# First head: one ScalarE table for squares and roots, centroids on ScalarE's queue, two wide copies of them, products of ones on TensorE meanwhile

## What is computed

```python
q_n = q / (norm(q) + 1e-6);  k_n = k / (norm(k) + 1e-6);  c_n = centroids / (norm(centroids) + 1e-6)
q_assign = argmax(einsum('bhsd,hcd->bhsc', q_n, c_n));  k_assign = argmax(einsum('bhsd,hcd->bhsc', k_n, c_n))
mask = q_assign[..., None] == k_assign[..., None, :]
scores = where(mask, q @ k.T / sqrt(64), -1e9)
attn = exp(scores - max) / (sum + 1e-9);  x = attn @ v
```

## Time and profile before

| | |
|---|---|
| median of 3 runs | 837.58 us (836.89 to 839.64) |
| the profiled execution | 838.31 us, its span 836.5 us |
| busy: PE, DVE, ACT, POOL | 802.8 (96%), 644.2 (77%), 493.5 (59%), 403.0 (48%) |
| transfers | 54.92 MB, mean 66 GB/s |

### The profile page before, as it was taken

One profiled execution on the slowest core, in us unless ns is written; L12 is line 12 of the kernel. 1 busy time (PEld: TensorE's weight loads), 2 busy tenths in 40 slices (PEclk: granted clock), 3 DMA queues, 4 the chain that ended last, 5 costly groups with the idle time before them and its releaser, 6 DMA issues.

```text
span 836.5 us, 15305 instructions
## 1 busy us (share of the span) xinstructions
PE 802.8 (96%) x5341; PEld 730.5 (87%) x5341; DVE 644.2 (77%) x1220; ACT 493.5 (59%) x895; POOL 403.0 (48%) x356
## 2 busy tenths in 40 slices
PE   4899999999999999999999999999999999999998
PEld 4798898888888879999899889898988999999997
DVE  4898898898898697665675667897767787878666
ACT  3778887887887668665555558878333222222221
POOL 0133543244567990760660663796194481919000
PEclk9999999999999999999999999999999999999999
DMA  6866645654732000010010010210020201100012
GB/s 136 186 154 146 132 105 134 148 113 104 161 91 66 20 27 26 26 51 26 26 51 26 26 52 15 63 51 2 26 63 1 76 1 52 38 26 26 36 40 77
DMA packets 65507, 54.92 MB, mean 66 GB/s; under 512 B 30112, under 2 KB 52640, under 8 KB 65440
## 3 DMA queue, kind: packets, MB, share of 16 engines
q1 hardware_dynamic: 65440, 54.06, 26.0%
HBM read 27.30 MB, written 3.15 MB: 36 GB/s over the span
## 4 chain that ended last, share of the span: by engine, by line
PE 79%; DVE 8%; issue 6%; ACT 5%; POOL 1%; DVEq 0%; DMA 0%; ACTq 0%; SPq 0%; POOLq 0%
PE ps L744 34%; PE ps L766 15%; PE ps L778 11%; PE ps L628 5%; PE ps L612 4%; PE ps L585 4%; PE ps L588 3%; DVE ptl L1306 2%; DVE sf L1297 2%; PE ps L656 1%; ACT pbuf L855 1%; PE ps L657 1%; ACT rsb L861 1%; ACT pth L845 1%; DVE hid L1433 0%
## 5 line engine op out<-in xcount | busy, mean ns | idle before, releaser
L744 PE MATMUL ps<-th,wh 128*128 128x256 f32 x840 | 239.6, 285 | 3.6 <-DVE pair L1401 1.2
L744 PE MATMUL ps<-tl,wh 128*128 128x256 f32 x840 | 237.6, 283 | 0.0
L744 PE MATMUL ps<-th,wl 128*128 128x256 f32 x840 | 237.6, 283 | 0.0
L744 PEld LDWEIGHTS ps<-th,wh 128*128 128x128 f32 x840 | 160.8, 191 | 8.7 <-DVE pair L1401 1.7
L744 PEld LDWEIGHTS ps<-tl,wh 128*128 128x128 f32 x840 | 160.9, 192 | 2.0
L744 PEld LDWEIGHTS ps<-th,wl 128*128 128x128 f32 x840 | 160.9, 192 | 0.0
L1297 DVE TENSOR_SCALAR_CACHE_REDUCE sf<-ps 128x768 f32<-128x768 f32 x96 | 91.3, 951 | 26.5 <-PE ps L588 25.4
L1832 POOL TENSOR_TENSOR wl<-wraw,wh 128x448 fp32r<-128x448 f32 x80 | 105.0, 1343 | 1.3
L845 ACT ACTIVATE pth<-ps 128x512 fp32r<-128x512 f32 x144 | 84.3, 589 | 29.4 <-PE ps L612 17.4
L855 ACT ACTIVATE pbuf<-sf,minn 128x768 f32<-128x768 f32 x96 | 89.6, 934 | 19.9 <-DVE sf L1297 19.8
L1306 DVE TENSOR_TENSOR ptl<-ps,pth 128x512 fp32r<-128x512 f32 x144 | 95.5, 682 | 3.9 <-ACT pth L845 3.8
(11 more groups left out here) (138 smaller groups left out, 1789.3 us busy)
## 6 DMA issues: line engine op xcount, KB each, us to landing
q<-atile SPq DMA_DIRECT2D x32, 192.0 KB, 3.3
k<-atile SPq DMA_DIRECT2D x32, 192.0 KB, 3.6
o1raw<-in_moe_w_out SPq DMA_DIRECT2D x8, 512.0 KB, 3.7
nat<-in_q SPq DMA_DIRECT2D x16, 192.0 KB, 3.9
nat<-in_k SPq DMA_DIRECT2D x16, 192.0 KB, 4.1
q<-btile SPq DMA_DIRECT2D x16, 192.0 KB, 3.2
k<-btile SPq DMA_DIRECT2D x16, 192.0 KB, 4.0
vnat<-in_v SPq DMA_DIRECT2D x16, 192.0 KB, 3.7
```

The lines of the kernel that those rows point to most:

```text
L744: last = pe.matmul(dst[:, 0:HC], a[w][:, j, kt, :], b[c][:, j, kt, :], start=(opened and kt == 0 and i == 0), stop=(kt == KH - 1 and i == ...
```

## The change

The centroids are loaded from ACT's queue, as ACT's first instruction. ACT then takes the root of the constant eps_c into an unused column of cst, before square and root of the centroids; it waits for the memset of eps_c only. The copies into cb are two instead of four, each over both batches at once with the source repeated, and so are DVE's subtractions; the first of these waits for the first copy alone. DVE fills eps_c and ones first and makes ident_r after the ramp. PE multiplies ones by ones into a bank of ps_s that nobody reads: 26 products before the transposition of ccat, 10 behind the transpositions of head 0's q and k in block -3. In block -3 the ranks (hits times ramp) are made by DVE behind the hits, and POOL leaves them out. In block -2 the transfer of stage into k2 is issued by ACT after its copy into stage; q2's stays on SP. The load of rmsg moves to block 0, in front of `load_up(0)`.

```diff
@@ sync
-            sp.dma_start(cnat[:, :], cent.rearrange("h c d -> (h c) d")).then_inc(centroids_loaded, 16)
...
-                    sp.dma_start(k2[D:D + NC, u].bitcast(F32), stage[NC:2 * NC, :].bitcast(F32)).then_inc(qk_assembled[u], 16)
+                    if fixed != -2:
+                        sp.dma_start(k2[D:D + NC, u].bitcast(F32), stage[NC:2 * NC, :].bitcast(F32))\
+                          .then_inc(qk_assembled[u], 16)
                 if fixed == 0:
+                    load_gain()
                     load_up(0)
@@ tensor
+            def warm(count):
+                for _ in range(count):
+                    pe.matmul(ps_s[:, 0, 0:P], ones[:, :], ones[:, :], start=True, stop=True)
+
+            pe.wait_ge(ones_made, 1)
+            warm(26)
             pe.wait_ge(ident_made, 2)
...
                     transpose_qk(n, u, fixed)
+                if fixed == -3:
+                    warm(10)
@@ scalar
+            act.dma_start(cnat[:, :], cent.rearrange("h c d -> (h c) d")).then_inc(centroids_loaded, 16)
+            act.wait_ge(root_ready, 1)
+            act.activation(cst[:, 4:5], eps_c[:, :], ACT.Sqrt)
             act.wait_ge(centroids_loaded, 16)
...
-            for i in range(4):
-                b, r = i // 2, i % 2
-                act.activation(cb[r * D:(r + 1) * D, b * H:(b + 1) * H, r * NC:(r + 1) * NC],
-                               ps_w[0][r * D:(r + 1) * D, 0, 0:P].rearrange("p (h c) -> p h c", h=H),
-                               ACT.Copy).then_inc(centroids_high, 1)
+            for r in range(2):
+                rows = slice(r * D, (r + 1) * D)
+                act.activation(cb[rows, :, r * NC:(r + 1) * NC].rearrange("p (b h) c -> p b h c", b=B),
+                               ps_w[0][rows, 0, 0:P].rearrange("p (h c) -> p h c", h=H).unsqueeze(1)
+                               .to_broadcast([D, B, H, NC]), ACT.Copy).then_inc(centroids_high, 1)
...
+                    if fixed == -2:
+                        act.wait_ge(mask_staged, 1)
+                        act.dma_start(k2[D:D + NC, u].bitcast(F32), stage[NC:2 * NC, :].bitcast(F32))\
+                           .then_inc(qk_assembled[u], 16)
@@ vector
+            dve.memset(eps_c[:, :], 1e-6).then_inc(root_ready, 1)
+            dve.memset(ones[:, :].bitcast(F32), 1.0).then_inc(ones_made, 1)
             for r, x in ((0, -float(D) ** -0.5), (1, 1.0)):
...
-            for i in range(4):
...
-                dve.wait_ge(centroids_high, 4)
...
+            for r in range(2):
+                rows = slice(r * D, (r + 1) * D)
+                dve.wait_ge(centroids_high, r + 1)
...
+                    if fixed == -3:
+                        dve.wait_ge(assignment_hits, 1)
+                        dve.tensor_tensor(eqr[:, :, :], eqb[:, :, :],
+                                          ramp[:, :].unsqueeze(1).to_broadcast([P, 2 * NT, NC]),
+                                          ALU.mult).then_inc(assignment_ranked, 1)
@@ gpsimd
-                if on(fixed, "asg"):
+                if on(fixed, "asg") and fixed != -3:
```

More of the change, by code:

```diff
@@ L187, in build @@
         ident_rounded = sem("ident_rounded")
+        root_ready = sem("root_ready")
+        ones_made = sem("ones_made")
         constants_made = sem("constants_made")
@@ L275, in slot_free @@
                     if pos % 4 < 2:
-                        eng.wait_ge(centroids_low, 4)
+                        eng.wait_ge(centroids_low, 2)
                     return
@@ L447, in _, with load_gain @@
             load_qk(0, 0, 0)
-            sp.dma_start(rmsg[:, :], rms_g.rearrange("(k p) -> p k", p=P),
-                         allow_slow_non_contiguous=True).then_inc(gain_loaded, 16)
+            def load_gain():
+                sp.dma_start(rmsg[:, :], rms_g.rearrange("(k p) -> p k", p=P),
+                             allow_slow_non_contiguous=True).then_inc(gain_loaded, 16)
             def load_up(q):
@@ L649, in assign @@
                     if fixed == -3:
-                        pe.wait_ge(centroids_low, 4)
+                        pe.wait_ge(centroids_low, 2)
                 s = (u + 1) % 2
@@ L1257, in _ @@
             dve.memset(half[:, :], 0.5)
[L1258 to L1261, removed]
             for c in range(NC):
@@ L1264, in _ @@
             dve.memset(minn[:, :, :], 0.0).then_inc(constants_made, 1)
+            dve.wait_ge(ident_made, 2)
+            dve.tensor_scalar(ident_r[:, :], ident[:, :], FAR_ROOT, None, ALU.mult).then_inc(ident_rounded, 1)
             dve.memset(cb[:, :, :].bitcast(F32), 0.0).then_inc(constants_made, 1)
@@ L1272, in _ @@
             dve.tensor_scalar(ccat[:, D:P], cnat[:, :], cst[:, 3:4], None, ALU.mult).then_inc(centroid_steps, 1)
-            for i in range(4):
-                b, r = i // 2, i % 2
-                dve.wait_ge(centroids_high, 4)
[L1276 to L1279, removed]
+            for r in range(2):
+                rows = slice(r * D, (r + 1) * D)
+                dve.wait_ge(centroids_high, r + 1)
+                dve.tensor_tensor(cb[rows, :, (2 + r) * NC:(3 + r) * NC].rearrange("p (b h) c -> p b h c", b=B),
+                                  ps_w[0][rows, 0, 0:P].rearrange("p (h c) -> p h c", h=H).unsqueeze(1)
+                                  .to_broadcast([D, B, H, NC]),
+                                  cb[rows, :, r * NC:(r + 1) * NC].bitcast(F32).rearrange("p (b h) c -> p b h c", b=B),
+                                  ALU.subtract).then_inc(centroids_low, 1)
             def second_t_lo(first, count):
```

## The result

The changed kernel takes 840.35 us (median of 20 runs, 838.91 to 844.15), the kernel before 838.32 (median of 20). The ratio is 1.0028, with a 95% interval of 1.0017 to 1.0039: 2.0 us slower, against a forecast of 835.2. The profiled execution took 840.32, its span 838.5.

The account below looks back on a forecast made before the run. TensorE was taken as the bound, 79% of the chain. Early rise 1.9 + 1.0 = 2.9, late 0.9 + 1.0 = 1.9; the middle, 2.4, gave 835.9 from the profiled execution, 835.2 against the median; 8-in-10 range 833.7 to 838.0.

Parts of the forecast that it names:

- The clock: At the start, the products of ones lift PE from 1.2 to 2.4 GHz; first scores' cuts gain 1.0 us in all.
- rise after 17 of the 26: The early rise: clock up at 4.8, the centroids' transposition at 5.8, 0.4 us earlier; 2.9 us gained in sum.
- rise at their end: The late rise: clock up when the 26 products end, transposition at 6.7, 0.5 us later; 1.9 us gained in sum.
- Rival 1: The early products of ones don't lift the clock; 0.4 us is left, 837.2; chance 0.22.
- no rise: Clock stays low at the start: btile at 9.4, 0.2 us later; first scores at 20.15, 0.4 earlier.
- The second rival: Clock rises, then falls back in PE's 3 us gap before the first scores; 836.2; chance 0.16.
- The 0.4 of the moved transfer: Before the first scores, k<-stage on ACT's queue lands beside q; without a rise, scores come 0.4 us earlier.
- rival 3: The clock rises later than now, low to 28 us; 2.7 more, less 0.4, 839.9 at most; chance 0.06.
- "Nothing" for the instructions themselves: Products of ones priced by PE's time alone: 26 take 5.5 us at 0.212; ten more hide in idle time.
- one for one behind 25 us: PE bounds the kernel from the first scores on, so a shift of the start carries unchanged to the end.
- the table: At the start, Square runs under Sqrt's table, one load; the transposition could start at 4.5, 1.7 us earlier.
- their 0.4: Ranks of the first assignment on DVE save 0.4 us, off the path unless the clock is low.

Follow-up runs that it names:

- e4: The changed kernel with 13 and 5 products of ones moving 512 columns in place of the 26 and 10 moving 128; 838.85 us, ratio 1.0007.
- e6: The kernel of e3 with 33 products of ones, 512 columns wide, in PE's gaps of the first two blocks; 838.85 us, ratio 1.0007.
- e14: The kernel of e2 with 64 tiny products of ones (50 and 14; 32 weight columns, 8 moved); 839.62 us, ratio 1.0012.
- e16: The changed kernel run once more, nothing edited, for a second profiled execution; 840.79 us, ratio 1.0034.
- e10: The changed kernel with 13 and 5 narrow products of ones in place of 26 and 10; 839.05 us, ratio 1.0000.
- after: The changed kernel itself, with the whole change; 840.35 us, ratio 1.0028 to the kernel before.
- e7: The kernel before with only the centroids' load on ACT's queue and the early root for one table load; 837.38 us, ratio 0.9988.
- e8: The changed kernel with its 36 products of ones made tiny (32 weight columns, 8 moved); 838.82 us, ratio 1.0005.
- e12: The kernel before with 36 tiny products of ones added at the changed kernel's places; 841.08 us, ratio 1.0030.
- e2: The changed kernel without its 36 products of ones, k2's transfer staying on ACT; 836.46 us, ratio 0.9977.
- e1: The changed kernel with the transfer of stage into k2 back on SP's queue; 840.28 us, ratio 1.0020.
- e3: The changed kernel without its products of ones and with k2's transfer back on SP; 836.88 us, ratio 0.9979.
- e15: The kernel before with 128 tiny products of ones added (90 and 38); 838.74 us, ratio 0.9999.

## Why the prediction was wrong

**The clock** is the step that failed, and with it the forecast: "rise after 17 of the 26" or "rise at their end". Rival 1 came instead. The products were 0.21 apart, as predicted for 1.2 GHz, for 9.3 us; the transposition came at 6.7 and btile at 9.4, the two numbers that the prediction gave for no rise, and the clock rose at 27.5 only. What stood against that rival, that 5.5 us are longer than the 2.1 us of the first assignment, was no reason: products four times as wide, in the same time, did it (e4). The second rival's outcome is real too: e4's clock rose and fell back, and e6's fell after the scores. But its mechanism, the gap of 3 us ahead of the first scores, isn't what did it: e4's clock fell at 12.25, with no gap over 1.09 between its rise and its fall. The Trainium skill's rule on idle gaps, cited there, doesn't explain that fall. Nor would the early rise have brought the forecast: in e4 it came at 5.4, and the median is 838.85.

**The 0.4 of the moved transfer.** Rival 1 was priced at 837.2 by k<-stage landing beside q at 20.15. It was issued beside q, at 17.61, but took 3.7 and landed behind it: the term is a loss of 0.1 to 0.5 by the scores' distance from btile (1.5 in e14), and in the changed kernel the first scores came 1.2 later than priced, 0.8 in e16. Vnat, priced at 3.9, took 4.7 and 4.2; q's 3.0 also stands against the 2.3 of the earlier trace rows. That the issue on ACT would be covered was right (0.62, and the first exponential wasn't late by it).

**A later rise: the small form of rival 3.** It was priced at 2.7, with "nothing but the missing rows" for it, as a case of 0.06. Its sign came, two scores products in 0.84 at 25.99; its price did not. The clock rose at 27.5, some 3 us later than before, and the cuts lost 0.6. The rise follows the first scores by 3.3 (e10) to 6.2 us (after), by 5.4 in e7 without any product and by 5.0 in e16, so it isn't carried with them, and the products alone don't set it; that price belongs in every case, with both signs.

**"Nothing" for the instructions themselves, and one for one behind 25 us.** The sum priced the products by PE's time alone. e8 and e12 have that time taken away and still lose 2.4 us against e2 and 2.5 (0.30%) against the kernel before. Of the 3.9 that the products cost in the changed kernel, some 1.5 are then left for the time in which they hold PE. The chain behind the start isn't rigid: a shift by 0.1 us between POOL and DVE turns 0.69 into 2.16. The step "a shift of the start carried to the end one for one" holds only for a kernel whose instructions lie where they lay: e2's first cut is 1.5 earlier, and its median 1.9 below the one before.

**Right:** the table. Square runs under Sqrt's table, there is one load, and without the products the transposition is at 4.13 (predicted 4.5). Two wide copies take 0.78, as predicted. The ranks are on DVE, and their 0.4 stay off the path: mask, stage and q<-stage come 0.1 earlier in spite of the later btile. And btile was the event to follow.

## What to carry to other kernels

An instruction that takes no time can cost some: before a time is put down to what an added instruction does, add as many that do next to nothing, and as many as fill a whole packet of the instruction queue. Where DVE and POOL run side by side, look in the profile for a DVE row at two or three times its usual length with a POOL row that started just ahead; such a pair, like a fall of TensorE's clock, sets executions of one kernel 1 to 3 us apart, and one profile shows only one draw; the mean granted clock of each run tells the second kind. Filler work for TensorE's clock is judged by the length of the products behind it, and for as long as the gaps last; and before anything is put into an empty stretch of an engine, ask what else in its queue could have used it, as the transposition did from 3.99 on.

## What the runs showed of the hardware

- 43 instructions of PE, busy 9.29 of 9.40 us with 128-column f32 products, left it at 1.2 GHz; 13 products of 512 columns, from 1.10 on, had it at 2.4 GHz by 5.4, read from their spacing.
- The clock fell back after it had been up in e1, e3, e6, e12, e15 and e16: between 25.5 and 33.1, for 3.4 to 10.2 us, at a cost of 1.1 to 1.7 us by the 17th cut against a late rise alone; and in e4 at 12.25, for 13.7 us. The two profiles of the kernel before show none of it, the mean clock of 56 of its 170 runs does.
- A transfer of 48 KB took 3.1 to 4.6 us from ACT's queue and 2.1 to 2.5 from SP's, issued 0.6 to 0.7 later (3.4 in e6, where both went out early). By landing they hardly differ: 0.31 to 0.69 and 0.27 to 0.50 behind q<-stage, e4 and e14 aside, and that just behind the 192 KB of vnat. Held copies did not change it.
- The table load at 1.18 took 1.28, as both had before, and cnat's issue on ACT 0.40, less than the 0.54 to 0.77 of the first ones on SP.
- The best version is e2: the change without its products, 836.46 and, again, 836.43. It beats both kernels, by 0.23% (0.08 to 0.39) and 0.17% (-0.01 to 0.35) against the kernel before.
